# Attention maxima in eleven pieces: 512-column tiles, and the short query tile over both halves of the keys at once

## What is computed

```python
B, H, S, D = q.shape            # 4, 8, 1152, 64
q_pool = q.reshape(B, H, S // 2, 2, D).mean(axis=3)
scores = scale * np.matmul(q_pool, k.transpose(0, 1, 3, 2))
scores = scores - np.max(scores, axis=-1, keepdims=True)
attn = np.exp(scores)
attn = attn / (np.sum(attn, axis=-1, keepdims=True) + 1e-09)
return np.matmul(attn, v)
```

## Time and profile before

| what | value |
|---|---|
| median of three runs | 1193.37 us (1192.91 to 1196.4) |
| the profiled execution, its own time | 1195.76 us |
| its span, first to last instruction | 1194.0 us, mean granted clock 0.993 |
| PE matmul busy | 1135.8 us, 95% of the span |
| PE weight loads (PEld) | 951.8 us, 80% |
| DVE busy | 651.6 us, 55% |
| ACT busy | 543.9 us, 46% |
| POOL busy | 523.4 us, 44% |
| reductions of line 647 | 465, 250.6 us busy, 556 ns each, 59.4 us of idle time before them |
| products of line 382 | 465, 166.0 us busy, 379 ns each |

### The profile page before, as it was taken

One profiled execution on the slowest core, in us unless ns is written; L12 is line 12 of the kernel. 1 busy time (PEld: TensorE's weight loads), 2 busy tenths in 40 slices (PEclk: granted clock), 3 DMA queues, 4 the chain that ended last, 5 costly groups with the idle time before them and its releaser, 6 DMA issues. The chain is left out here.

```text
span 1194.0 us, 19539 instructions
## 1 busy us (share of the span) xinstructions
PE 1135.8 (95%) x7232; PEld 951.8 (80%) x7232; DVE 651.6 (55%) x1370; ACT 543.9 (46%) x1131; POOL 523.4 (44%) x560
## 2 busy tenths in 40 slices
PE   6999999989999999997899999789999999999998
PEld 5777777777777778786777777489898989899896
DVE  5888877877888888866556565553121212122120
ACT  4666666556666666546565656633110201111110
POOL 6888899998888888734333333300000000000000
PEclk9999999999999999998999999999999999999999
DMA  8222111221111221002001010142100001010000
GB/s 205 61 60 61 56 46 51 60 60 46 51 55 60 60 60 41 22 27 115 2 1 41 1 45 24 40 146 62 53 1 27 27 1 53 0 53 0 27 1 27
DMA packets 47559, 54.56 MB, mean 46 GB/s; under 512 B 10992, under 2 KB 29424, under 8 KB 46960
## 3 DMA queue, kind: packets, MB, share of 16 engines
q1 hardware_dynamic: 46864, 53.12, 14.4%
q10 hardware_dynamic: 608, 0.30, 0.1%
HBM read 43.97 MB, written 9.44 MB: 45 GB/s over the span
## 5 line engine op out<-in xcount | busy, mean ns | idle before, releaser
L647 DVE TENSOR_REDUCE part_max<-psA 128x1 f32<-128x384 f32 x465 | 250.6, 556 | 59.4 <-PE psA L382 36.7
L576 ACT ACTIVATE pT<-psA 128x576 f32<-128x576 f32 x288 | 187.9, 653 | 165.5 <-PE psA L401 156.4
L270 POOL TENSOR_TENSOR pT<-pT 128x576 f32<-128x576 f32 x157 | 225.3, 1435 | 26.2 <-ACT pT L576 4.3
L382 PE MATMUL psA<-kT,qT 128*128 128x384 f32 x465 | 166.0, 379 | 11.5 <-DVE part_max L647 11.1
L415 PE MATMUL psA<-pT,v_raw 128*64 128x288 f32 x1152 | 153.8, 412 | 0.0
L1770 ACT ACTIVATE hid_hi<-psC 128x384 fp32r<-128x384 f32 x96 | 47.2, 492 | 198.7 <-PE psC L1695 198.6
L392 PE MATMUL psA<-qT,kT 128*128 128x288 f32 x576 | 132.2, 311 | 0.0
L1789 DVE SCALAR_TENSOR_TENSOR hid_lo<-psC,hid_hi 128x384 fp32r<-128x384 f32 x96 | 53.5, 558 | 137.9 <-ACT hid_hi L1770 137.9
L401 PE MATMUL psA<-qTm,kT 128*128 128x288 f32 x576 | 123.0, 295 | 0.5 <-ACT qTm L562 0.5
L415 PEld LDWEIGHTS psA<-pT,v_raw 128*64 128x64 f32 x1152 | 77.0, 136 | 53.2 <-issue 6.4
L1711 PE MATMUL psC<-w_hi,hid_hi 128*128 128x512 f32 x288 | 113.5, 394 | 0.0
(11 more groups left out here) (165 smaller groups left out, 1948.2 us busy)
## 6 DMA issues: line engine op xcount, KB each, us to landing
k_raw<-in_k SPq DMA_DIRECT2D x32, 288.0 KB, 2.9
v_raw<-in_v SPq DMA_DIRECT2D x32, 288.0 KB, 2.8
q_raw<-in_q SPq DMA_DIRECT2D x31, 256.0 KB, 3.3
w_raw<-in_moe_w_ch SPq DMA_DIRECT2D x1, 4096.0 KB, 12.3
u_rows<-x_all SPq DMA_DIRECT2D x16, 256.0 KB, 2.0
w_raw<-in_moe_w_ch SPq DMA_DIRECT2D x16, 256.0 KB, 2.6
u_first<-u_rows SPq DMA_DIRECT2D x3, 768.0 KB, 4.5
u_second<-u_rows SPq DMA_DIRECT2D x3, 768.0 KB, 4.7
```

What stands on the lines that cost most here:

```text
L270: nc.gpsimd.tensor_tensor(pT[:, KT, :], pT[:, KT, :], pT[:, j, :], ALU.add).then_inc(part_summed, 1)
L382: nc.tensor.matmul(maxes[n % 2][:, 0:PIECE], qT[h % 3][:, t * P:(t + 1) * P], kT[u][:, c * PIECE:(c + 1) * PIECE], start=True, stop=True). ...
L576: nc.scalar.activation(pT[:, j, :].rearrange("p (a c) -> p a c", a=2), scores[n % 2][:, :, 0:HALF], ACT.Exp, scale=0.5 * float(D) ** -0.5) ...
L647: nc.vector.tensor_reduce(part_max[u][:, t, c:c + 1], maxes[n % 2][:, 0:PIECE], AX.X, ALU.max).then_inc(max_freed[n % 2], 1)
```

## The change

The maxima of a head are cut into eleven pieces. Two groups of four pieces are one full query tile each against 512 keys ("a": keys 0 to 511, "b": 512 to 1023). Piece "c" holds the last 128 keys against all four full query tiles, as four matmuls of 128 columns in one bank, reduced by one instruction to four numbers. The short tile of 64 queries stands twice in `qT`, which grows from 640 to 768 columns: at 512 (rows 0 to 63 of a product) and at 640, so that the 128 columns from 576 on are 64 zeros and the 64 queries. Two matmuls that accumulate then give the 64 queries against the first 576 keys on partitions 0 to 63 and against the other 576 on partitions 64 to 127. This goes in two pieces, "half" 0 with 512 columns (two matmuls) and "half" 1 with 64 (two matmuls). `maximum` first copies the two maxima of the upper 64 partitions beside those of the lower ones with a DVE copy of 64 x 2 numbers, waits for it (`halves_moved`), and then reduces over four columns rather than three. The columns that stay unused hold `LOWEST`, written once at the start. ACT's copy of the short tile writes 256 columns rather than 128.

```diff
-    PIECES = ([(t, c) for c in range(2) for t in range(QT - 1)] + [(QT - 1, 0), (QT - 1, 1)]
-              + [(t, 2) for t in range(QT)])
+    PIECES = ([("a", t) for t in range(QT - 1)] + [("b", t) for t in range(QT - 1)]
+              + [("c", None), ("half", 0), ("half", 1)])
+    HALF_KEYS = S // 2
+
 
     TURN_USES = [("ka", 0), ("kb", 0), ("kc", 0), ("ka", 1), ("kb", 1)]
...
-        qT = [sb(f"qT{u}", [P, WIDE], F32R) for u in range(3)]
+        qT = [sb(f"qT{u}", [P, WIDE + P], F32R) for u in range(3)]
         qTm = [sb(f"qTm{u}", [P, WIDE], F32R) for u in range(2)]
-        part_max = [sb(f"part_max{u}", [P, QT, 3]) for u in range(2)]
+        part_max = [sb(f"part_max{u}", [P, QT, 4]) for u in range(2)]
         pT = sb("pT", [P, KT + 1, SQ])
         p_sum = sb("p_sum", [P, SQ])
...
+        halves_moved = sem("halves_moved")
         padded = sem("padding_written")
         k1_zeroed = sem("k1_rows_zeroed")
...
-        PADS = 8
+        PADS = 10
 
...
-                u, (t, c) = h % 2, PIECES[at]
+                u, (kind, t) = h % 2, PIECES[at]
                 n = max_no(h, at)
+                out, q, k = maxes[n % 2], qT[h % 3], kT[u]
                 if at == 0:
                     pe.wait_ge(qa_copied, h + 1)
-                for first, name in (((0, 0), "ka"), ((0, 1), "kb"), ((QT - 1, 0), "kc")):
-                    if (t, c) == first:
+                for first, name in ((("a", 0), "ka"), (("b", 0), "kb"), (("c", None), "kc")):
+                    if PIECES[at] == first:
                         pe.wait_ge(turn_freed, keys_before[name, h] + 1)
                 if n >= 2:
                     pe.wait_ge(max_freed[n % 2], n // 2)
-                nc.tensor.matmul(maxes[n % 2][:, 0:PIECE], qT[h % 3][:, t * P:(t + 1) * P],
-                                 kT[u][:, c * PIECE:(c + 1) * PIECE], start=True, stop=True
-                                 ).then_inc(max_filled, 1)
+                if kind == "half":
+                    a, z = ((0, BANK), (BANK, HALF_KEYS))[t]
+
+                    parts = [(out[:, 0:z - a], q[:, c:c + P],
+                              k[:, m * HALF_KEYS + a:m * HALF_KEYS + z])
+                             for m, c in enumerate(((QT - 1) * P, SQ))]
+                elif kind == "c":
+                    parts = [(out[:, t * P:(t + 1) * P], q[:, t * P:(t + 1) * P], k[:, 2 * BANK:S])
+                             for t in range(QT - 1)]
+                else:
+                    at = 0 if kind == "a" else BANK
+                    parts = [(out, q[:, t * P:(t + 1) * P], k[:, at:at + BANK])]
+                for m, (to, queries, keys) in enumerate(parts):
+                    mm = nc.tensor.matmul(to, queries, keys, start=kind != "half" or m == 0,
+                                          stop=kind != "half" or m == 1)
+                mm.then_inc(max_filled, 1)
 
             def score(h, j):
...
                 if more2:
                     turn_queries(h + 2)
+                score(h, 3)
                 maxima(4, 5)
-                score(h, 3)
+                if h > 0:
+                    turn_out(h - 1)
                 maxima(5, 6)
                 if h > 0:
-                    turn_out(h - 1)
+                    sum_rows(h - 1)
                 maxima(6, 7)
-                if h > 0:
-                    sum_rows(h - 1)
+                score(h, 4)
                 maxima(7, 8)
-                score(h, 4)
+                values(h, range(EARLY))
                 maxima(8, 9)
-                values(h, range(EARLY))
-                maxima(9, 11)
                 score(h, 5)
-                maxima(11, 12)
+                maxima(9, 10)
                 if more2:
                     turn_keys(h + 2, "ka", range(0, 4))
-                maxima(12, 13)
                 score(h, 6)
-                maxima(13, 14)
+                maxima(10, 11)
                 score(h, 7)
-                maxima(14, 15)
                 score(h, 8)
                 if more2:
...
-                    nc.scalar.activation(qT[h % 3][:, 4 * P:WIDE], turn[:, P:2 * P], ACT.Copy)
+                    nc.scalar.activation(
+                        qT[h % 3][:, 4 * P:].rearrange("p (n c) -> p n c", c=P),
+                        turn[:, P:2 * P].unsqueeze(1).to_broadcast([P, 2, P]), ACT.Copy)
                     ins = nc.scalar.activation(kT[u][:, 8 * P:S], turn[:, 0:P], ACT.Copy)
...
-                u, (t, c), n = h % 2, PIECES[at], max_no(h, at)
+                u, (kind, t), n = h % 2, PIECES[at], max_no(h, at)
+                src = maxes[n % 2]
                 dve.wait_ge(max_filled, n + 1)
-                nc.vector.tensor_reduce(part_max[u][:, t, c:c + 1], maxes[n % 2][:, 0:PIECE],
-                                        AX.X, ALU.max).then_inc(max_freed[n % 2], 1)
+                if kind == "half":
+                    to = part_max[u][:, QT - 1, t:t + 1]
+                    src = src[:, 0:BANK if t == 0 else HALF_KEYS - BANK]
+                elif kind == "c":
+                    to = part_max[u][:, 0:QT - 1, 2]
+                    src = src.rearrange("p (t k) -> p t k", k=P)
+                else:
+                    c = 0 if kind == "a" else 1
+                    to = part_max[u][:, t, c:c + 1]
+                nc.vector.tensor_reduce(to, src, AX.X, ALU.max).then_inc(max_freed[n % 2], 1)
 
             def wide_maxima(t):
                 dve.wait_ge(wide_filled, t + 1)
-                nc.vector.tensor_reduce(part_max[0][:, t, :], wide(t), AX.X, ALU.max
+                nc.vector.tensor_reduce(part_max[0][:, t, 0:3], wide(t), AX.X, ALU.max
                                         ).then_inc(wide_reduced, 1)
...
                 else:
-                    dve.wait_ge(max_freed[n % 2], n // 2 + 1)
+                    for m in (n - 1, n):
+                        dve.wait_ge(max_freed[m % 2], m // 2 + 1)
+
+                    nc.vector.tensor_copy(part_max[u][0:LAST, QT - 1, 2:4],
+                                          part_max[u][LAST:P, QT - 1, 0:2]
+                                          ).then_inc(halves_moved, 1)
+                    dve.wait_ge(halves_moved, h)
                 nc.vector.tensor_reduce(q_lo_m[u][:, :, D], part_max[u][:, :, :], AX.X, ALU.max,
                                         negate=True).then_inc(m_ready, 1)
...
             nc.vector.memset(oT[:, HALF + SHIFT:3 * P], 0.0).then_inc(padded, 1)
+            nc.vector.memset(part_max[0][:, :, 3:4], LOWEST).then_inc(padded, 1)
+            nc.vector.memset(part_max[1][:, :, 2:4], LOWEST).then_inc(padded, 1)
             nc.vector.memset(group_sums[:, SQ // BLOCK:], 0.0).then_inc(padded, 1)
...
             for h in range(HEADS - 1):
                 for at in range(len(PIECES)):
-                    if at == 9 and h > 0:
+                    if at == 8 and h > 0:
                         normalise(h - 1)
```

More of the change, by code:

```diff
@@ L30 @@
 MASKED = -1000000000.0
+LOWEST = -3.0e38
 def ceil_div(a, b):
```

## The result

The changed kernel takes 1202.4 us (median of six runs, 1201.21 to 1204.15) against 1194.92 for the kernel before in the same comparison (six runs, 1192.91 to 1196.88). The ratio is 1.0063, 95% interval 1.0052 to 1.0075: slower by 7.5 us, beyond the 0.3% that could pass for no change, and 1.4 above the top of the range given. The forecast was no change, so it was wrong.

The account below looks back on a forecast made before the run. PE was taken to bound the outer stretches and POOL the middle one; 0.03 us a head on 22 heads, 0.7 us, turned the median of 1193.37 into 1192.7. The range was 1184 to 1201.

Parts of the forecast that it names:

- What bounds the kernel: Attention: PE sets the pace in the outer stretches, POOL in seven middle heads; the change acts fully on 22 heads.
- Columns and loads: PE in a head: 5760 columns before and after, 2.40 us; short matmuls 0.12 each, piece "c" 0.50, "half" 1 0.25.
- The start of the early values: PE, first part of a head: DVE just keeps up; values start at 5.94 and end 0.20 later than before.
- Tile 8: PE, late in a head: tile 8 waits for the exponent of tile 6 and starts at 11.30.
- just fit: ACT before the exponent of tile 6: its copy of the turned keys, 0.60, ends about 10.6, in time.
- Sum: Whole kernel: 0.03 us a head gained on 22 heads, 0.7 us; no measurable change had chance 0.38.
- The load price: Slower rival, PE: each of six short matmuls waits for its whole load, 0.19; 0.28 a head, 1199.6 us; chance 0.17.
- 0.15 more of waits behind `sum_rows` gone: Far end of the faster rival (chance 0.38), PE before the values: all gains together 0.41 a head, 1184.4 us.
- The copy as a bottleneck: Slower rival, DVE: the copy meets POOL's next add and delays the maximum; 1.1 a head, 1217 us; chance 0.07.

Follow-up runs that it names:

- e8: e3 with piece "c" as one matmul of 512 columns and "half" 1 as one of 128, giving wrong maxima: 1189.43 us, ratio 0.9961 to the kernel before.
- e1: The changed kernel with piece 4 of the maxima ahead of the scores of tile 3 again: 1198.75 us, ratio 1.0033 to the kernel before.
- e4: The changed kernel with reductions of "a" and "b" reading 256 of 512 columns, leaving out keys: 1193.36 us, ratio 0.9988 to the kernel before.
- e3: The changed kernel with both moves, those of e1 and e2: 1192.11 us, ratio 0.9974 to the kernel before.
- e2: The changed kernel with the first turning of keys and ACT's copy of it behind tile 6's scores and exponent: 1196.7 us, ratio 1.0013.
- e7: e3 without the DVE copy and its wait, leaving out some maxima: 1193.93 us, ratio 0.9993 to the kernel before.
- e6: The kernel before the change, with its first turning of keys and ACT's copy of it moved behind tile 6: 1201.11 us, ratio 1.0054.

## Why the prediction was wrong

**What bounds the kernel: right.** The loss lies in the two stretches in which PE is the bound, 0.29 for each head; the middle one was to take 119 to 120 and took 118.60, a little less. Nothing of DVE's relief came through by itself.

**Columns and loads: right in the main.** Piece "c" took 0.50 from start to tile 5, as forecast; "half" 0 0.47 (0.46), the turned keys 0.29 (0.30), the last turnings 0.82 (0.80), the late values 2.57 (2.57). "half" 1 was priced too high, 0.14 for 0.25, and that was hidden. The scores of tile 5, behind the four short matmuls, took 0.58 for 0.53. The forecast charges such an uncovered load to tile 6 behind the short turnings, but not here; with "c" as one matmul (e8) tile 5 took 0.54. The Trainium skill (TensorE: Matmul & The Clock Gate, on the back-to-back issue gap) has 81 ns between such matmuls, by which "c" is estimated 0.15 shorter. This trace does not agree: the loads of "c" and the load behind them stand 0.11 apart (four from 368.44 to 368.88), and with the first one uncovered the piece took 0.50.

**The start of the early values: the step that failed.** "In the new order piece n + 2 may start 0.74 after piece n + 1 could, and 0.76 is what a score tile and a piece take: DVE just keeps up, so I remove 0.1 and add 0.05". The values were to start at 5.94 and started at 6.17. This compares two rates, and takes DVE to be working without a gap from piece 0 on. A reduction cannot begin before its piece is there, and the diff put piece 4 behind the scores of tile 3. It starts at 3.80, DVE stands idle for 0.44 until it can reduce it, and piece 6 has to wait for that reduction: 0.44 + 0.68 + 0.07 = 1.19 from the start of piece 4, in which PE has only 0.93 of its own work, the turned output, piece 5 and `sum_rows` (0.80 to 364.78, and 0.13). The 0.26 that is missing is the wait, and the 0.20 to 0.22 that e1 takes away again. With piece 4 in its old place (e1) the values start at 5.97, the number of the forecast to 0.03, but not by its working: e4 shows that the price of DVE in the kernel before was near 0.2, not 0.1, and that 0.15 of it remains, not 0.05. Two errors of 0.1 cancel there, which is luck.

**Tile 8: right in size, and not seen as a loss.** The forecast had it 1.47 behind tile 6, held by the exponent; it was 1.51, of which 0.04 more because the copy of keys did not "just fit": it ended at 371.08, some 0.06 to 0.1 after the exponent could have begun. I entered this wait as a fact of the kernel. But it had grown by the change: before, PE had two pieces of 384 columns and tile 7 between tile 6 and tile 8, and tile 8 came 1.45 behind tile 6, just when the exponent ended. Now PE has only "half" 1 and tile 7 there, and its own work is 1.36 (0.60, 0.14, and 0.62 for a tile 7 with no wait behind it, as in e3) where the exponent takes 1.51; and the load behind the wait is uncovered, 0.1 more. e2 puts the turning of 0.29 between tile 6 and tile 8, and gets back 0.26 in the second part. Without that the second part had gained 0.12 of the 0.38 that e3 shows.

**Sum.** The forecast of a head was 15.30 and it is 15.62: 0.23 at the values, 0.05 at tile 5, 0.04 at tile 8, 0.02 at the turnings, less 0.01 in the early values: 0.33 for the head shown. Times 22 heads that is 7.3. Forecast was a gain of 0.7 and measured a loss of 7.5, so 8.2 are to be explained; the 0.9 that is left lies within the interval of the ratio, 1.3 to 1.4 to either side.

**The rivals.** The load price (1199.6) came nearest with its total, by a wrong mechanism: "c" would have been 0.81, and it was 0.50. The range missed for a reason of its own: the price of DVE's waits was varied on the side of gains alone ("0.15 more of waits behind `sum_rows` gone"), never as a new wait. The copy as a bottleneck did not come about: forecast "near 11.6" for its end, measured 11.72 (371.90), and PE wanted the maximum 0.6 after it was there. That POOL's add holds it is borne out:

```profile
370.45 1.43 POOL L277 TENSOR_TENSOR pT<-pT 128x576 f32<-128x576 f32 x1 [0.21 <-ACT pT L596]
```

This add ends at 371.88, the copy at 371.90. In 22 heads of the changed kernel (copies from 49.92 to 159.23 and from 293.45 to 496.49) the copy takes 0.35 and ends 0.02 to 0.03 behind the add that runs as it starts; in nearly all such heads of e3 it takes 0.48, at the same distance; where it meets no running add (174.85, in a head in which POOL is the bound) it takes 0.17. The Trainium skill (SBUF — State Buffer, on who interferes with whom) says that copies of VectorE can take the port pair shared with GpSimd and are then blocked for the whole of its running instruction; the copies here, of 128 numbers each, agree: 0.35 us in the head shown and 0.73 in e8, each to the end of an add. The rival that was lacking is the one that won: the reordered pieces arrive in bunches, so that DVE idles first and PE waits next.

**What stays open.** Why e7's ratio is above e3's, in so far as it is more than spread, and what delayed DVE's addition in two of its heads. The order is not searched either: e8 says that some 0.1 more a head is to be had where PE has fewer loads, but it does not compute the maxima, and a piece "c" with one load would need the queries as the moving operand, which was not tried.

## What to carry to other kernels

Where two engines hand each other two buffers in turn, comparing their rates is not enough. Walk the loop from each piece to its reduction and to the piece that reuses the buffer, with the start of each: an idle stretch of the second engine in the middle was not made up here. When a change takes work out of the faster engine's list, the work left on the slower one has to be spread again, because what was removed may have covered another latency (here ACT's exponent, between two score tiles). And try a reordering that comes with a change of shapes by itself: from the kernel before to e3 a head changed by -0.16, from e3 to the changed kernel, by the order alone, by +0.45. No order was best for both: the place of the turning that helped the new pieces cost the old ones 0.28 (e6).

## What was not expected of the hardware

- A matmul that has waited on a semaphore costs more here than the wait. Its load starts with it (both at 371.79) instead of ahead of it: from tile 8 to the turning behind it is 0.63 after the wait (371.79 to 372.42) and 0.53 without one (365.43 to 365.96 in e3).
- A reduction begins 0.43 to 0.44 after the start of a 512-column matmul that it waits for (360.81 to 361.24, 363.98 to 364.42), while PE spends some 0.23 on such a matmul (0.47 for the two from 369.52 to 369.99). So a loop through both engines has about 0.2 in it in which neither does work for it.
- Moving 0.3 us of PE work by one score tile cost the kernel before 0.28 a head (e6), and gained 0.22 in the changed kernel (e2).
